# Attention and two MLPs: the first product of each MLP as one level of Strassen, and one MLP after the other

## What is computed

```python
# q, k, v: (1, 6016, 256)
qn = q / (np.linalg.norm(q, axis=1, keepdims=True) + 1e-06)
kn = k / (np.linalg.norm(k, axis=1, keepdims=True) + 1e-06)
a = softmax(kn.transpose(0, 2, 1) @ qn / tau)     # (1, 256, 256)
x = (v @ a)                                       # 6016 tokens, 256 channels
h = x @ w1_in                                     # 256 -> 2048
x2 = (h * sigmoid(1.702 * h)) @ w1_out            # 2048 -> 256
h = x2 @ w2_in
out = (np.maximum(h, 0) + alpha * np.minimum(h, 0)) @ w2_out
```

## Time and profile before

| what | value |
|---|---|
| time, median of 3 runs (lowest to highest) | 1108.68 us (1108.28 to 1110.57) |
| span of the profiled execution | 1106.9 us |
| PE (TensorE matmul) busy | 1098.3 us, 99% |
| DVE busy | 623.9 us, 56% |
| ACT busy | 405.2 us, 37% |
| POOL busy | 29.4 us, 3% |

### The profile page before, as it was taken

How to read it: one execution, slowest core, us unless ns; L and a number is a source line. 1 busy time by engine, 2 the same in 40 slices (tenths; PEclk the granted TensorE clock), 3 DMA queues, 4 the chain that set the end, 5 groups by cost and what they waited for, 6 DMA issues and landing times.

```text
span 1106.9 us, 13843 instructions
## 1 busy us (share of the span) xinstructions
PE 1098.3 (99%) x4937; PEld 912.6 (82%) x4937; DVE 623.9 (56%) x954; ACT 405.2 (37%) x715; POOL 29.4 (3%) x28
## 2 busy tenths in 40 slices
PE   9999999999999999999999999999999999999998
PEld 8899898888888888888888888888888888888886
DVE  6974474275276257258348437527626725834775
ACT  6785523323323323322432432332332332343221
POOL 4500000000000000000000000000000000000000
PEclk9999999999999999999999999999999999999999
DMA  8742000010010110110100100001001011010011
GB/s 338 271 118 77 0 1 15 1 20 10 10 20 0 19 19 0 19 19 0 19 14 5 19 5 14 14 5 19 5 14 19 0 19 19 0 19 0 1 20 20
DMA packets 108536, 33.37 MB, mean 30 GB/s; under 512 B 100048, under 2 KB 104672, under 8 KB 108256
## 3 DMA queue, kind: packets, MB, share of 16 engines
q1 hardware_dynamic: 30368, 23.34, 6.7%
q10 hardware_dynamic: 78144, 9.71, 5.7%
HBM read 26.88 MB, written 6.16 MB: 30 GB/s over the span
## 4 chain that ended last, share of the span: by engine, by line
PE 98%; DMA 1%; DVE 0%; SPq 0%; ACT 0%; issue 0%
PE ps L308 32%; PE ps L309 32%; PE ps L310 32%; PE ps L401 2%; DMA q_sb<-q_dram 1%; PE ps L435 0%; PE ps L439 0%; PE ps L436 0%; DVE inv_norm L732 0%; SPq L259 0%; DVE sim L735 0%; SPq L260 0%; DVE neg_max L737 0%; DVE out_sb L680 0%; ACT sim L539 0%
## 5 line engine op out<-in xcount | busy, mean ns | idle before, releaser
L618 DVE TENSOR_TENSOR g_lo<-g,g_hi 128x512 fp32r<-128x512 f32 (+1 forms) x384 | 259.6, 676 | 341.0 <-ACT g_hi L477 331.2
L482 ACT ACTIVATE g_hi<-g 128x512 fp32r<-128x512 f32 (+1 forms) x192 | 119.7, 623 | 400.4 <-DVE g L638 400.4
L474 ACT ACTIVATE g<-ps 128x512 f32<-128x512 f32 (+1 forms) x192 | 113.1, 589 | 275.9 <-PE ps L310 275.9
L634 DVE TENSOR_SCALAR neg_part<-ps,alpha_T 128x512 f32<-128x512 f32 (+1 forms) x192 | 141.9, 739 | 125.4 <-PE ps L310 125.4
L308 PE MATMUL ps<-g_hi,w1o_hi 128*128 128x512 f32 (+1 forms) x384 | 150.1, 391 | 0.0
L309 PE MATMUL ps<-g_lo,w1o_hi 128*128 128x512 f32 (+1 forms) x384 | 150.1, 391 | 0.0
L310 PE MATMUL ps<-g_hi,w1o_lo 128*128 128x512 f32 (+1 forms) x384 | 150.0, 391 | 0.0
L308 PE MATMUL ps<-g_hi,w2o_hi 128*128 128x512 f32 (+1 forms) x384 | 148.0, 385 | 0.0
L309 PE MATMUL ps<-g_lo,w2o_hi 128*128 128x512 f32 (+1 forms) x384 | 147.9, 385 | 0.0
L310 PE MATMUL ps<-g_hi,w2o_lo 128*128 128x512 f32 (+1 forms) x384 | 147.9, 385 | 0.0
L308 PE MATMUL ps<-vT_hi,w1i_hi 128*128 128x512 f32 (+1 forms) x352 | 136.8, 389 | 0.0
(11 more groups left out here) (106 smaller groups left out, 1053.3 us busy)
## 6 DMA issues: line engine op xcount, KB each, us to landing
k_sb<-k_dram SPq DMA_DIRECT2D x10, 512.0 KB, 11.5
q_sb<-q_dram SPq DMA_DIRECT2D x10, 512.0 KB, 13.2
out_dram<-out_sb ACTq DMA_DIRECT2D x76, 64.0 KB, 1.9
v_raw<-v_dram ACTq DMA_DIRECT2D x72, 64.0 KB, 2.0
stage<-w_in_dram SPq DMA_DIRECT2D x4, 512.0 KB, 13.5
w1o_raw<-w_out_dram SPq DMA_DIRECT2D x1, 2048.0 KB, 8.6
stage<-w_in_dram SPq DMA_DIRECT2D x1, 2048.0 KB, 9.2
stage<-w_out_dram SPq DMA_DIRECT2D x1, 2048.0 KB, 8.3
```

The lines of the kernel that those rows point to most:

```text
L474: nc.scalar.activation(g[:, f % 2, 0:n], ps[:, H + f % NH, 0:n], ACT.Gelu_apprx_sigmoid)
L482: nc.scalar.activation(g_hi[:, f % NG, 0:n], g[:, f % 2, 0:n], ACT.Copy).then_inc(hi_ready, 1)
L618: return nc.vector.tensor_tensor(lo, full, hi.bitcast(fp32), ALU.subtract)
L634: nc.vector.tensor_scalar(neg_part[:, f % 2, 0:n], h, 0.0, alpha_T[:, f:f + 1], ALU.min, ALU.mult).then_inc(neg_done, 1)
```

## The change

For a pair of token tiles (t = 0, 1) and a pair of hidden chunks (i = 0, 1) the first product is a 2 by 2 block product (over the two halves of the 256 input channels). It took 8 block products; now it takes 7, by the Strassen-Winograd scheme, from sums and differences of weight blocks and of input blocks. A block product is still three matmuls.

- Tiles are pairs: `PAIRS` = 6, the first pair with two tiles of 448 tokens, the others of 512. A step `n` is one of `QUADS` = 8 pairs of hidden chunks of one pair of tiles. There are 48 steps for the first MLP (`LAYER`) and then 48 for the second. A step is 7 block products of its own (`top`, 21 matmuls) and the second products of the step before (`second`, 24 matmuls), interleaved by hand.
- The first MLP runs over all tokens first. Its result goes to DRAM (`x2_stash`) and is loaded again in the second half. The second MLP's weights are loaded, summed and split late in the first half.
- Partial results share PSUM banks: products 1, 6, 7, 4 accumulate in bank `Y(n)` and are copied out by ACT in between (`keep`); 2 goes to `X`; 5, then 3 on top, to `Z`. DVE adds bank and kept copy (`sum_block`). The outputs take four banks.
- The activation is made over: ACT applies Gelu once and copies once (`activate`, `high`), DVE subtracts (`low_block`). In the second MLP ACT makes relu(-h) and DVE adds (1 - alpha) times it (`leak`).
- Sums of input blocks (`tops_1`, `tops_23`, `tops_4`) and of weight blocks (`wide_tops`, `wi_tops`) and the `lo` halves of the weights (`wide_lows`, `wi_lows`) are POOL's. Those of the very first weight blocks are DVE's.
- `turn_order` gives the order in which `second` takes the four blocks; it differs in the first and the last step of a pair. `take_out` empties the output banks at the border of two pairs.
- All loads and stores are on SP. The loops are written out (no `Fori`).

The core of the diff:

```diff
+        PRODUCT = {1: (0, 0), 2: (1, 5), 3: (6, 2), 4: (2, 6), 5: (3, 1), 6: (4, 3), 7: (5, 4)}
...
+        def turn_order(n):
+            return (G11, G21, G22, G12) if n % QUADS in (0, QUADS - 1) else (G11, G22, G21, G12)
...
+        def store(sp, gp):
+            p = gp % PAIRS
+            for t in range(2):
+                for c in range(KC):
+                    sp.wait_ge(y_out, 4 * gp + 2 * t + c + 1)
+                    at, nt = token(p, t), half(p)
+                    if gp < PAIRS:
+                        sp.dma_start(x2[c, :, at:at + nt], out_sb[:, 2 * t + c, 0:nt]).then_inc(stored, 16)
+                        continue
+                    for i in range(NQ):
+                        sp.dma_start(out_v[i, c, :, at // Q:(at + nt) // Q, :],
+                                     out_sb[i * Q:(i + 1) * Q, 2 * t + c, 0:nt].rearrange("s (b r) -> s b r", r=Q)).then_inc(stored, 16)
...
+            def tops_23(gp):
...
+                pool.wait_ge(x_tops, 4 * gp + 1)
+                pool.wait_ge(x_low, TOPS * gp + B11 + 1)
+                minus(x_raw[:, 0, 0:nt], x_raw[:, 2, 0:nt], x_raw[:, 4, 0:nt]).then_inc(x_tops, 1)
+                minus(x_raw[:, 1, 0:nt], x_raw[:, 2, 0:nt], x_raw[:, 1, 0:nt]).then_inc(x_tops, 1)
...
+            for fb in range(NFB):
+                pool.wait_ge(w0_high, fb * KC + 2)
...
+                minus(w0_lo[:, 1, cols], stage[:, 1, cols], w0_hi[:, 1, cols].bitcast(fp32)).then_inc(w0_pool, 1)
+                if fb == 1:
+                    tops_1(0)
+                if fb == 2:
+                    tops_23(0)
+                    tops_4(0)
...
+            def wide_lows(fb):
+                pool.wait_ge(wide_high, fb + 1)
+                s = slice(2 * fb, 2 * fb + 2)
+                minus(wi_lo[:, s], wide[:, fb, :, 0:TOPS, :], wi_hi[:, s].bitcast(fp32)).then_inc(wide_low, 1)
...
+            def step(n):
+                if n < STEPS:
...
+                    top(1, n, Y(n), True)
+                if n > 0:
+                    second(n - 1, 0, 4)
+                    pe.wait_ge(c_ready[G22], n)
+                    top(3, n - 1, Z, False)
+                    second(n - 1, 4, 7)
+                if n < STEPS:
+                    pe.wait_ge(p1_kept, n + 1)
+                    top(6, n, Y(n), False)
+                if n > 0:
+                    second(n - 1, 7, 11)
+                if n < STEPS:
+                    if n > 0:
+                        pe.wait_ge(c_ready[G11], n)
+                    top(2, n, X, True)
+                if n > 0:
+                    second(n - 1, 11, 14)
+                if n < STEPS:
+                    pe.wait_ge(u2_kept, n + 1)
+                    top(7, n, Y(n), False)
+                if n > 0:
+                    second(n - 1, 14, 18)
+                if n < STEPS:
+                    if n > 0:
+                        pe.wait_ge(c_ready[G12], n)
+                    top(5, n, Z, True)
+                if n > 0:
+                    second(n - 1, 18, 21)
+                if n < STEPS:
+                    pe.wait_ge(u3_kept, n + 1)
+                    top(4, n, Y(n), False)
+                if n > 0:
+                    second(n - 1, 21, 24)
...
+            def high(n, b):
+                nt = width(n)
+                if layer(n) == 0:
+                    act.wait_ge(acted[b], n + 1)
+                else:
+                    act.wait_ge(leaky[b], n - LAYER + 1)
+                if n > 0:
+                    act.wait_ge(y_used[b], n)
+                copy(g_hi[:, b, 0:nt], g[:, b, 0:nt]).then_inc(g_high[b], 1)
+
+            for n in range(STEPS + 1):
...
+                if n < STEPS:
+                    keep(n, 0, 1, p1_kept)
+                if n > 0:
+                    high(n - 1, G21)
+                    activate(n - 1, G12)
+                if n < STEPS:
+                    keep(n, 1, 6, u2_kept)
+                if n > 0:
+                    high(n - 1, G12)
...
+                if n in (0, 2, 3):
+                    wide_part({0: 1, 2: 2, 3: 3}[n])
...
+                activate(n, G11)
+                keep(n, 2, 7, u3_kept)
+                high(n, G11)
...
+                activate(n, G22)
+                activate(n, G21)
+                high(n, G22)
...
+            def sum_block(n, b):
...
+                product, bank, kept = {G11: (2, X, 0), G22: (5, Z, 2), G12: (3, Z, 1)}[b]
+                dve.wait_ge(p_done[product], n + 1)
+                dve.wait_ge({G11: p1_kept, G22: u3_kept, G12: u2_kept}[b], n + 1)
+                nc.vector.tensor_tensor(g[:, b, 0:nt], part[:, kept, 0:nt], ps[:, bank, 0:nt], ALU.add).then_inc(c_ready[b], 1)
...
+            def leak(n, b):
...
+                dve.wait_ge(acted[b], n + 1)
+                nc.vector.scalar_tensor_tensor(out=g[:, b, 0:nt], in0=below[{G11: 1, G22: 0, G21: 1, G12: 0}[b]][:, 0:nt],
+                                               scalar=rest_T[:, f:f + 1], in1=ps[:, Y(n), 0:nt] if b == G21 else g[:, b, 0:nt],
+                                               op0=ALU.mult, op1=ALU.add).then_inc(leaky[b], 1)
...
+            for n in range(STEPS + 2):
+                gp, s = pair(n) + 1, n % QUADS
+                if s == 1 and n > 1:
+                    take_out(gp - 2, 1, 0)
+                    take_out(gp - 2, 1, 1)
+                if n > 0:
+                    low_block(n - 1, G22)
+                    sum_block(n - 1, G12)
+                    if layer(n - 1) == 1:
+                        low_block(n - 1, G21)
+                        leak(n - 1, G12)
+                    else:
+                        low_block(n - 1, G21)
+                if n < STEPS:
+                    sum_block(n, G11)
+                if n > 0:
+                    low_block(n - 1, G12)
+                if n < STEPS:
+                    if layer(n) == 1:
+                        leak(n, G11)
...
+                    if n < QUADS - 1:
+                        wo_part(n + 1)
...
+                    sum_block(n, G22)
+                    low_block(n, G11)
...
+                    if layer(n) == 1:
+                        leak(n, G22)
+                        leak(n, G21)
+                if s == 0 and n > 0:
+                    take_out(gp - 2, 0, 0)
+                    take_out(gp - 2, 0, 1)
```

More of the change, by code:

```diff
@@ new lines, in attention_mlp_mlp, with Y @@
+        wi_raw = place("wi_raw", [P, 8, P], fp32, R + 168 * KB)
+        ps = ctx.enter_context(nc.psum_tensor("ps", [P, 8, BANK], fp32))
+        H = 4
+        X, Z = 6, 7
+        def Y(n):
+            return H + n % 2
+        PRODUCT = {1: (0, 0), 2: (1, 5), 3: (6, 2), 4: (2, 6), 5: (3, 1), 6: (4, 3), 7: (5, 4)}
+        A21 = 7
+        B11, T1, B22, T2, T3, B21, T4 = range(TOPS)
+        G11, G12, G21, G22 = range(4)
+        BLOCK = {G11: (0, 0), G12: (0, 1), G21: (1, 0), G22: (1, 1)}
@@ L203, in attention_mlp_mlp @@
         PIECES = KC * FF // WP
[L204 removed]
+        W0_UNDER = next(n + 1 for n, (j, nb) in enumerate(CHUNKS) if (j + nb) * C >= KC * FF)
         W0_LOADS = 4
@@ new lines, in second @@
+            def second(n, begin, end):
+                nt, s, gp = width(n), n % QUADS, pair(n)
+                order = turn_order(n)
+                for m in range(begin, end):
+                    b = order[m // 6]
+                    c, kind = divmod(m % 6, 3)
+                    i, t = BLOCK[b]
+                    f = 2 * s + i
+                    if m == 0 and n % LAYER < QUADS:
+                        pe.wait_ge(wo_low, layer(n) * QUADS + s + 1)
+                    if m % 6 == 0:
+                        pe.wait_ge(g_low[b], n + 1)
+                    opens = s == 0 and b in (G11, G22)
+                    if opens and kind == 0 and gp > 0:
+                        pe.wait_ge(y_out, 4 * (gp - 1) + 2 * t + c + 1)
+                    closes = s == QUADS - 1 and b in (G21, G12)
+                    wh, wl = wo_hi[:, f, c * P:(c + 1) * P], wo_lo[:, f, c * P:(c + 1) * P]
+                    done = nc.tensor.matmul(ps[:, 2 * t + c, 0:nt], wl if kind == 2 else wh, (g_lo if kind == 1 else g_hi)[:, b, 0:nt],
+                                            start=opens and kind == 0, stop=closes and kind == 2, skip_group_check=True)
+                    if m % 6 == 5:
+                        done.then_inc(y_used[b], 1)
+                    elif closes and m % 6 == 2:
+                        done.then_inc(y_half, 1)
@@ new lines, in _ @@
+            act.wait_ge(inv_ready, 1)
+            widen(0)
+            widen(1)
+            x_part(0, B11)
+            split_w0(3)
+            x_part(0, T1)
+            widen(2)
+            widen(3)
+            wide_part(0)
+            x_part(0, B22)
+            x_part(0, T2)
+            widen(4)
+            widen(5)
+            x_part(0, T3)
+            x_part(0, B21)
+            widen(6)
+            widen(7)
+            x_part(0, T4)
+            load_table(ACT.Gelu_apprx_sigmoid)
```

870 lines of the change are left out of this document (429 added, 441 removed).

## The result

The changed kernel takes 1143.05 us, median of 4 runs (1140.09 to 1146.89), the kernel before 1108.63 us beside it: a ratio of 1.0307, 95% interval 1.0284 to 1.0331, so 3.1% slower. The forecast was 1112 us with a range of 1095 to 1126. The direction it held likeliest was right; the size was wrong by 31 us, and the time lies outside the range.

A forecast was written before the change was run, and what follows sets the result against it. PE's matmul work was taken as the bound. The span of 1106.9 us, less 64.9, plus 37.6 (borders), 23.2 (start), 5.2 (end) and 2.0 (collisions), gave 1110.0, plus 1.8 around it: 1112 us, range 1095 to 1126.

The forecast's parts named there:

- fewer columns: Every step: 45 matmuls instead of 48, 144,384 columns fewer at 0.449 ns each, -64.9 us, bounds 60 to 66.
- start, up to step 8: Start: POOL and DVE collisions delay step 1's end by 17.2 us, steps 2 and 3 by 3.0 each: +23.2 us.
- borders, 21 outside start and change of MLP: Borders of pairs: G21's rest stands behind G12's sum on DVE, stalling PE 1.22 to 2.73 us each; +33.6 us here.
- change of MLP: two borders: Two border stalls of the same kind, at the change from first to second MLP: +3.95 us.
- change of MLP: weights: Loading and preparing the second MLP's weights late in the first half costs nothing, since a load lands in some step: 0.
- end: End: one queue issues 16 stores, so the span ends 10.5 us after the last matmul: +5.2 us, 3 to 6.
- mid-run collisions: Mid-run: POOL's input sums, four a pair, collide with DVE, mostly in slack: +2 us, bounds 0 and 10.
- a rival of 0.10: Start: PE's idling drops the granted clock for 78 matmuls up to step 1's end, some 10 us: 1122; chance 0.10.
- The fast start: Start: POOL and DVE overlap better or long subtractions are let through, so it costs 10.3 us: 1099; chance 0.38.
- POOL did not reach into ordinary steps of the second MLP: Second MLP: POOL's 1.28 us operations land ahead of G22's subtraction, ten steps pay 1.3, ten 0.2: 1127; chance 0.12.
- my four cases: Whole kernel: forecast 1105 to 1118 (0.40), fast start 1099 (0.38), POOL in second MLP 1127 (0.12), clock 1122 (0.10).
- the ring: Not forecast; change of MLP: ACT's w2_in split, POOL's subtraction, SP's loads, ACT's w2_out split wait in turn, steps 16 to 17 us.

The follow-up runs named there:

- experiment 2: Changed kernel without loading, summing and splitting the second MLP's weights, its products using the first MLP's: 1108.62 us.
- experiment 1: Changed kernel with the load of a w2_out piece ahead of the wait for a split w2_in piece in SP's list: 1126.56 us.
- experiment 5: Changed kernel with w2_out's load ahead on SP (1126.6 us), plus POOL's second-MLP weight work ahead of its sums of input blocks: 1123.21 us.
- experiment 6: Changed kernel with PE's three long waits of the start filled with 27, 12 and 10 small matmuls on a free bank: 1139.98 us.
- Experiment 9: Kernel with all mends together (1086.9 us), plus waits in steps 0 and 1 filled with small matmuls and POOL's second-pair sum T1 moved ahead: 1086.23 us.
- experiment 7: Changed kernel with POOL's subtraction of 1792 columns cut into four of 384 and 512 columns: 1138.12 us.

## Why the prediction was wrong, step by step

**What failed** is one sentence of the part on mid-run work: "The stash, its loads, the second MLP's weights: nothing; a step is 10 us, a load lands in some". It counted the work of each engine and not what stands behind each wait on SP and ACT. Measured, the weights cost 38.0 us (experiment 2), more than the whole miss of 31. Of these 19.6 go by the order of two loads on SP (200.6 - 181.0 in the traces, experiment 1) and 3.5 more by POOL's order (experiment 5). The rest, 15 us, was not divided further, and its causes are read from the trace and not shown by a run: steps of 10.8 instead of 10.2, the wait of 3.2 us at the first `take_out` of the second MLP, and `wo_part` in lists already full of leaks.

A second step failed beside it: the start was summed at the full clock. Its waits were forecast as 23.2 us and are 20.8; the 9.8 us of slower matmuls had no term.

**The sum, term by term** (span, in us):

| term | forecast | measured |
|---|---|---|
| fewer columns | -64.9 | -72.6 |
| start, up to step 8 | +23.2 | +31.2 |
| borders, 21 outside start and change of MLP | +33.6 | +28.9 |
| change of MLP: two borders | +3.95 | +3.35 |
| change of MLP: weights | 0 | +38.0 |
| end | +5.2 | +3.6 |
| mid-run collisions; measured: what is left over | +2.0 | +3.0 |
| sum with 1106.9 | 1110.0 | 1142.4 |

- Columns: a regular pair of tiles of the first MLP took 84.09 us with 2.18 of gaps, so (84.09 - 2.18)/360 = 0.2275 us a matmul; of the second (85.80 - 3.43)/360 = 0.2288. By the mean, 0.4456 ns a column, 2,165,760 columns take 965.2 us against 1037.8. I had carried over 0.449.
- Borders: the mechanism held in each of its parts. The row has gaps alone; the restart (0.33 us instead of 0.23 from 333.06 to 333.39) lies in the measured price of a column. With it a border costs 1.19 us for 1.22 forecast, and 1.19 for 1.31. In the second MLP's second step the two gaps are 1.04 (banks) and 1.31 (G21), with restarts 2.55 for 2.73. The forecast had the banks' wait within G21's; it stands by itself.
- Start: the chain was followed well: PE's seventh group at 66.8 (forecast 67.9), first copy at 75.2 (74.1), second product at 85.3 (84.05). From step 0 to step 8 the undisturbed end would be 132.9, the gap came at 164.1: 31.2. (Undisturbed, 76.4 was 0.6 too high: step 0 has 18 matmuls and not 21, its product 3 stands in step 1.) The waits are smaller than forecast: steps 2 and 3 cost 2.2 and 3.3 us for 3.0 each, and the one of step 3 is also a wait for a place in SBUF, which the forecast didn't have. What made the start dearer is the clock, that I had set aside as a rival of 0.10.
- End: the 16 stores on one queue took 8.54 us as forecast, the span ended 8.9 us after the last matmul (5.3 before), not 10.5.

The SP queue at the end, and the last matmul:

```profile
1132.06 8.54 SPq L243 DMA_DIRECT2D out_dram<-out_sb  x16
```

```profile
1133.25 0.39 PE L433 MATMUL ps<-g_hi,wo_lo 128*128 128x512 f32 x1
```

**The rivals.** The fast start was not there. POOL did not reach into ordinary steps of the second MLP: 786 to 872 us shows the border gaps alone. The clock did fall, on top of the forecast and not in its place. Its slower matmuls take 9.8 us in the start, close to the rival's 10; filling the first waits gave back 3.9 (experiment 6). In the change of MLP it fell again (0.82 and 0.86 above). The Trainium skill (TensorE: Matmul & The Clock Gate, "Why this matters for your kernels") warns against idle gaps of PE, and the trace agrees: 0.43 us a matmul behind the 6.5 us wait, 0.23 when that wait is filled. Experiment 9 adds that a fill is worth nothing where other waits take up what it gains. None of my four cases had the ring; together they held all of the chance and ended at 1127 at most, which left no room for it.

The rule of the Trainium skill that was weighed (VectorE: DVE Perf Modes, "The DRAIN you can't avoid") would have made the borders longer. The two DVE operations at 331.71 and 332.31 start 0.60 apart and last 0.69. The same section says that a next operation that is not held starts earlier, which the prediction left out; the 0.60 us go with that.

**Whether Strassen pays.** Yes, when nothing waits for it: 1082.3 us is 2.4% below the kernel before. That is 26.7 us of the 65 to 73 which fewer columns give. In its trace PE's gaps over 0.33 us add up to 13 us in the start, 13 in the change of MLP and 6 at later borders, which is most of the rest. The reloaded weights come from running one MLP after the other, not from Strassen; no run tries the one without the other.

## What to carry to other kernels

When work is rare, such as reloading weights between two phases, don't price it by its engine time but follow one turn of it: which wait stands ahead of the load in the queue's list, and what stands behind the instruction that takes the loaded piece. A split of a late piece in the middle of ACT's list held up a whole step four times, by 2.4 to 4.0 us each. Buffers laid over one another are waits too, and the profile names them only by the engine that frees the place.

Follow each list against the positions of the engine that bounds, as was done for the borders: it gave their gaps of 1 to 2.5 us to within 0.2. In the start it gave waits of 23.2 us where 20.8 were measured, but not what the clock adds behind a long wait.

## What was not expected of the hardware

A DVE subtraction of two SBUF tiles ends only after POOL's operation beside it: 0.69 us became 2.73 (81.38 to 84.11) beside one from 79.55 to 83.57; with POOL's cut in pieces of 384 and 512 columns, 0.9 to 1.0 (experiment 7). POOL's 1792 columns took 4.0 to 4.1 us in one operation, 4.44 in four, and 5.3 in four with DVE at work beside them. The same matmul of 512 columns came every 0.230 us on average before and every 0.2275 to 0.2288 after, restarts included; no run here shows why. Holding the granted clock at 1.00 gained 3.9 us in experiment 6 and nothing in experiment 9.
